# RWKV-style attention and two feed-forward layers on one core: where the decay test and its two small inputs are handled

## The chip, the cores and the metric

The kernel runs on 1 core of a Trainium2 chip. The metric is the device time of one execution in microseconds (us); the figure compared is the median over several runs. The core has a matrix engine (TensorE, PE in the profile), VectorE (DVE), ScalarE (ACT), GpSimd (POOL) and SyncE (SP), each with its own instruction stream; they wait for each other by semaphores. Loads and stores are DMAs, issued by an engine on its own queue and carried out by 16 DMA engines that all queues share. In this kernel SyncE issues all loads, and ScalarE's queue is used for stores only.

## The reference, cut to what matters

Shapes: B=4, H=8, S=768, D=48, so 3072 tokens of width 384. All is float32.

```python
# attention: r, k, v [B,H,S,D]; decay w [H,D]; bonus u [H,D]
for t in range(S):
    cur = einsum('bhd,bhe->bhde', u * k_t, v_t)
    y[t] = einsum('bhd,bhde->bhe', r_t, state + cur)
    state = w * state + einsum('bhd,bhe->bhde', k_t, v_t)
# layer 1 (384 -> 1536 -> 384):  ((x @ w_a) * (x @ w_b)) @ w_out
# layer 2 (384 -> 2048 -> 384):  h = x @ w_in;  (h * clip(h + 3, 0, 6) / 6) @ w_out
```

The inputs have w between 0.85 and 0.95.

## The kernel before, in words

**The whole.** The attention is done in 24 chunks of 128 steps of one batch (`CH = 128`, six tiles of four batches). In a chunk, r and k are multiplied by powers of w and of 1/w, so that the recurrence becomes matrix products. This is safe only for w in a range, 0.75 to 1.33; therefore the kernel tests the range on the chip and holds two complete paths, a fast one and a general one. The four chunks of tile 0 are done in a prologue; all later ones beside the matrix products of layer 1. Then layer 2 follows. The products of both layers are done as three products of high and low parts each (`PRODUCTS`), with weights cut into those parts by ScalarE and GpSimd while TensorE works. The orders of all engines are written out by hand, by slots (`slot_a`, `slot_b`, `slot_d`).

**The prologue, engine by engine.** SyncE (`first_loads`, L387) issues w_u_col (the pairs of w and u, 5 KB), then `first_rk` of chunks 0 to 3 (r and k turned, 512 KB each), then two loads of v. After the flag it goes on with the loads of the fast path (`sync_fast`). VectorE (`guard_and_tables`, L1184) sets `zeros` and the first power, waits for w_u_col, compares w with the lower and the upper bound (L1196, L1198), computes the powers of w by four scans (L1201), then compares the count that TensorE has made (L1204), casts it to the integer flag (L1206), makes the reciprocals (L1208, L1209), waits for `first_rk` of chunk 0 and multiplies its r and k (`first_product`, L1049), makes the table of 1/w powers (L591), and goes on with the chunks (`scale` L1044, `mask` L1067 and L1072). GpSimd sets `three`, makes the masks by eight selects (`make_masks`, L478, the select itself is L487), zeroes the state (L1270) and reads the flag. ScalarE loads its function table with its first activation (L1279), reads the flag, and copies and scales for the chunks (L1002, L854). TensorE multiplies zeros (`keep_warm`, L756, 4 or 2 blocks of 128 columns), sums `in_range` times 3 into the count (L1293), multiplies zeros again (4 blocks and then 2), and begins the chunks (`first_chunks`): `own_of_first` (L630) needs the product of chunk 0, ScalarE's copies (L1002, L854) need `own_of_first`, and VectorE's first mask (L1067) needs ScalarE's copies.

**The flag.** Each engine but TensorE calls `decide`: wait for the flag, read it, branch.

Of the kernel before, what the change touches and what calls it, by code (L numbers as in the profile page):

```python
# [20 lines left out]
ALU = mybir.AluOpType  # L21
ACT = mybir.ActivationFunctionType
AX = mybir.AxisListType

P = 128
# [13 lines left out]
W_MIN, W_MAX = 0.75, 1.33  # L39
# [8 lines left out]
def build(nc, r, k, v, w, u, w_a, w_b, w_out, w_in2, w_out2, rk_turned, natural, w_u_pairs, outT):  # L48
# [11 lines left out]
    NP = H // 2  # L60
    W2 = HP + D
# [17 lines left out]
    with ExitStack() as ctx:  # L79
        def sb(name, shape, dt=F32, of=ctx, align=None):  # L80
            if align:
                return of.enter_context(nc.sbuf_tensor(name, shape, dt, align_bytes=align))
            return of.enter_context(nc.sbuf_tensor(name, shape, dt))
# [5 lines left out]
        acc_ps = ctx.enter_context(nc.psum_tensor("acc_ps", [P, KC, TOK], F32))  # L89
        att_ps = ctx.enter_context(nc.psum_tensor("att_ps", [P, 3, TOK], F32))  # L90
# [16 lines left out]
        with ExitStack() as setup:  # L107

            in_range = sb("in_range", [P, NP], of=setup)
            all_in = sb("all_in", [1, 1], of=setup)  # L110
            inv_fine = sb("inv_fine", [P, NP, FINE + 1], of=setup)
            inv_coarse = sb("inv_coarse", [P, NP, COARSE + 1], of=setup)
            zeros = sb("zeros", [P, CH], of=setup)
            tab_sT = sb("tab_sT", [P, NP, CH], of=setup)
# [5 lines left out]
        flag = sb("flag", [1, 1], I32)  # L120


        with ExitStack() as att:
# [4 lines left out]
            w_u_col = sb("w_u_col", [P, 3, NP], of=att)  # L128
# [12 lines left out]
        s_guard, s_count, s_flag = sem("guard_chain"), sem("in_range_counted"), sem("flag_ready")  # L141
        s_w_u, s_u_all, s_masks = sem("w_and_u_loaded"), sem("u_for_all_loaded"), sem("masks_made")
# [26 lines left out]
        s_three = sem("three_set")  # L169
# [135 lines left out]
        def x_view(tile, z, q):  # L305
            return x_cut[:, tile % 2, z, :, cols_of(q)]

        count_ps = acc_ps[0:1, 1, 0:1]
        HD = H * D
        by_head = lambda x: x.rearrange("s (h d) -> s h d", h=H)  # L310
        A_of = lambda q: first_A[:, q % 2] if 2 <= q < B else A[:, q % 2]
# [73 lines left out]
                         x2T_v[:, :, t * TOK:(t + 1) * TOK]).then_inc(s_x2_loaded, 16)  # L385

        def first_loads(sp):  # L387
            sp.dma_start(w_u_col[0:W2], w_u_pairs).then_inc(s_w_u, 16)
            load_first_rk(sp, 0)
            load_first_rk(sp, 1)  # L390
            load_first_rk(sp, 2)
            load_first_rk(sp, 3)
            load_first_v(sp, 0)
            load_first_v(sp, 1)
# [80 lines left out]
                sp.dma_start(outT_v[:, j, cols], st[:, j, :]).then_inc(s_st, 16)  # L475


        def make_masks(pool):  # L478


            def keep_where(at, rows, column, row, base, times, compare):

                block = masks_sb[rows, at:at + times * MID]
                if times > 1:
                    block = block.rearrange("s (n t) -> s n t", n=times)
                pattern = [[column, MID]] if times == 1 else [[0, times], [column, MID]]
                nc.gpsimd.affine_select(out=block, in_=block, pattern=pattern, compare_op=compare, fill=0.0,  # L487
                                        base=base, channel_multiplier=row).then_inc(s_masks, 1)

            every, low_half, high_half = slice(0, P), slice(0, MID), slice(MID, P)  # L490
            late = 2 * P + MID
            nc.gpsimd.memset(masks_sb[:], 1.0).then_inc(s_ones, 1)
            pool.wait_ge(s_ones, 1)
            keep_where(0, every, 1, -1, 0, 1, ALU.is_equal)
            keep_where(MID, every, 1, -1, MID, 1, ALU.is_equal)
            keep_where(P, every, 1, -1, MID, 1, ALU.is_equal)
            keep_where(P + MID, every, 1, -1, 0, 1, ALU.is_equal)
            keep_where(2 * P, low_half, 1, -1, 0, 1, ALU.is_gt)
            keep_where(late, every, 1, -1, MID, NP // 2, ALU.is_gt)
            keep_where(late + NP // 2 * MID, low_half, 1, -1, 0, NP // 2, ALU.is_gt)  # L500
            pool.wait_ge(s_masks, MASK_PARTS - 1)
            keep_where(2 * P, high_half, 1, -1, 0, 1, ALU.is_gt)
            pool.wait_ge(s_masks, MASK_PARTS)
# [250 lines left out]
        def keep_warm(pe, times, bank=up_ps[:, 1]):  # L754

            pe.matmul(bank[:, 0:times * CH].rearrange("p (n c) -> p n c", n=times), zeros[:],  # L756
                      zeros[:].unsqueeze(1).to_broadcast([P, times, CH]), start=True, stop=True)
# [423 lines left out]
                    if i == 4 and t + 1 < TILES:  # L1181
                        x2_low(dve, t + 1)

        def guard_and_tables(dve):  # L1184

            links = [0]

            def link(ins):
                links[0] += 1
                ins.then_inc(s_set, 1)  # L1190

            link(dve.memset(zeros[:], 0.0))
            link(dve.memset(power[:, :, 0:1], 1.0))
            dve.wait_ge(s_set, links[0])
            dve.wait_ge(s_w_u, 16)
            dve.tensor_scalar(in_range[0:W2], w_col[0:W2], W_MIN, None, ALU.is_ge).then_inc(s_guard, 1)  # L1196
            dve.wait_ge(s_guard, 1)
            dve.scalar_tensor_tensor(out=in_range[0:W2], in0=w_col[0:W2], scalar=W_MAX, in1=in_range[0:W2],  # L1198
                                     op0=ALU.is_le, op1=ALU.mult).then_inc(s_guard, 1)
            for p in range(NP):  # L1200
                link(dve.tensor_tensor_scan(power[0:W2, p, 1:CH + 1], w_col[0:W2, p:p + 1].to_broadcast([W2, CH]),  # L1201
                                            zeros[0:W2, :], 1.0, ALU.mult, ALU.add))
            dve.wait_ge(s_count, 1)
            dve.tensor_scalar(all_in[:], count_ps, 3.0 * W2 * NP - 1.0, None, ALU.is_ge).then_inc(s_guard, 1)  # L1204
            dve.wait_ge(s_guard, 3)
            dve.tensor_copy(flag[:], all_in[:]).then_inc(s_flag, 1)  # L1206
            dve.wait_ge(s_set, links[0])
            link(dve.reciprocal(inv_fine[0:W2], fine[0:W2]))  # L1208
            link(dve.reciprocal(inv_coarse[0:W2], coarse[0:W2]))  # L1209
            first_product(dve, 0)  # L1210
            dve.wait_ge(s_set, links[0])
            table(dve, tab_rk[0:W2, 1, :, 0:CH], inv_coarse[0:W2, :, 0:COARSE],
                  inv_fine[0:W2, :, 1:FINE + 1]).then_inc(s_tabT, 1)
# [37 lines left out]
        def decide(eng):  # L1251
            eng.wait_ge(s_flag, 1)
            return eng.value_load(flag[0:1, 0:1], min_val=0, max_val=1)

        with nc.Block() as block:
            @block.sync
            def _(sp):
                first_loads(sp)
                flag_sp = decide(sp)
                with sp.If(flag_sp == 1):  # L1260
                    sync_fast(sp)
                with sp.Else():
                    sync_general(sp)
                store_last(sp)
                sp.wait_ge(s_st, 16 * (2 * TILES - 1 + KC))
            @block.gpsimd
            def _(pool):
                nc.gpsimd.memset(three[:], 3.0).then_inc(s_three, 1)
                make_masks(pool)
                nc.gpsimd.memset(state[:], 0.0).then_inc(s_zero, 1)  # L1270
                flag_pool = decide(pool)
                with pool.If(flag_pool == 1):
                    pool_fast(pool)
                with pool.Else():
                    pool_general(pool)
            @block.scalar
            def _(act):
                act.wait_ge(s_three, 1)
                nc.scalar.activation(first_use[:], three[:], ACT.Copy)  # L1279
                flag_act = decide(act)  # L1280
                with act.If(flag_act == 1):
                    scalar_fast(act)
                with act.Else():
                    scalar_general(act)
                evacuate_last(act)
            @block.tensor
            def _(pe):
                pe.wait_ge(s_set, 1)
                keep_warm(pe, 4)
                pe.wait_ge(s_three, 1)  # L1290
                pe.wait_ge(s_guard, 2)
                for p in range(NP):
                    mm = pe.matmul(count_ps, in_range[0:W2, p:p + 1], three[0:W2, :], start=(p == 0), stop=(p == NP - 1))  # L1293
                mm.then_inc(s_count, 1)
                keep_warm(pe, 4)
                keep_warm(pe, 2)
                first_chunks(pe)
                tensor_layer1(pe)
                tensor_layer2(pe)
            @block.vector  # L1300
            def _(dve):
                guard_and_tables(dve)
                flag_dve = decide(dve)
                with dve.If(flag_dve == 1):
                    vector_fast(dve)
                with dve.Else():
                    vector_general(dve)
# [172 lines left out]
```

## Time and profile before

| | us |
|---|---|
| median of 3 runs | 919.6 (919.18 to 920.41) |
| profiled execution, device time | 919.12 |
| its span, first to last instruction | 917.3 |
| TensorE busy | 911.9 (99%) |
| VectorE, ScalarE, GpSimd busy | 369.5, 329.5, 184.3 |
| mean granted TensorE clock | 1.00 |

The profiled execution's device time is 1.8 us over its span. Times of instructions are counted from the span's start. An entry "idle before <- X" says what an engine waited for. A start time and a busy time of a merged group do not have to add up to the next start, since neighbours overlap by the engine's pipeline.

### The profile page before, as it was taken

The page shows a single profiled execution, that of the slowest core. Times are in us where ns is not written, and L with a number is a line of the kernel's source. Part 1 is how long each engine was busy: PE and PEld are TensorE (multiplying, and loading weights), DVE is VectorE, ACT ScalarE, POOL GpSimd, SP SyncE. Part 2 cuts the span into 40 slices and gives each one's busy share as a digit, 9 for nine tenths or more (in the row PEclk, how much of TensorE's full clock was granted, in tenths as well). Part 3 has the DMA queues.
Part 4 walks back from the last instruction along what each step waited for, and adds up shares of the span by engine and source line. Part 5 has one row for each costly group of instructions (what it writes and reads, how often), then busy time and mean ns, then how long its engine had stood idle before and what let it go on. Part 6 is the DMA issues. An engine that isn't in the chain of part 4 may idle for free.

```text
span 917.3 us, 15108 instructions
## 1 busy us (share of the span) xinstructions
PE 911.9 (99%) x6400; PEld 746.4 (81%) x6400; DVE 369.5 (40%) x607; ACT 329.5 (36%) x651; POOL 184.3 (20%) x168
## 2 busy tenths in 40 slices
PE   8999999999999999999999999999999999999998
PEld 6788888888888888888888888888888888888887
DVE  7746344525443343334222343343343343343332
ACT  6645323232333233242221343433333333333333
POOL 5976102111111111010755570000000000000000
PEclk9999999999999999999999999999999999999999
DMA  8653211121120121131311210100200100100000
GB/s 307 198 167 108 90 50 62 55 90 56 56 110 34 56 110 55 38 129 48 115 50 55 78 50 1 65 5 1 69 1 0 70 1 7 64 0 1 35 1 36
DMA packets 24281, 57.84 MB, mean 63 GB/s; under 512 B 2320, under 2 KB 8080, under 8 KB 24208
## 3 DMA queue, kind: packets, MB, share of 16 engines
q1 hardware_dynamic: 19808, 48.18, 15.6%
q10 hardware_dynamic: 4400, 8.65, 2.5%
q8 instruction: 50, 0.82, 0.4%
q14 instruction: 23, 0.19, 0.1%
HBM read 47.39 MB, written 9.44 MB: 62 GB/s over the span
## 4 chain that ended last, share of the span: by engine, by line
PE 98%; DVE 1%; DMA 0%; ACT 0%; issue 0%; SPq 0%; DVEq 0%; ACTq 0%
PE up_ps L722 32%; PE up_ps L799 21%; PE acc_ps L736 16%; PE acc_ps L813 11%; PE att_ps L813 11%; PE att_ps L614 2%; PE att_ps L677 1%; PE att_ps L682 1%; PE att_ps L646 1%; PE att_ps L663 1%; PE att_ps L671 1%; DMA first_rk<-in_rk_turned 0%; ACT A L854 0%; DVE first_rk L1044 0%; DVE first_A L1067 0%
## 5 line engine op out<-in xcount | busy, mean ns | idle before, releaser
L722 PE MATMUL up_ps<-x_cut,w_up 128*128 128x512 f32 x1296 | 307.3, 391 | 0.2 <-ACT x_cut L867 0.2
L722 PEld LDWEIGHTS up_ps<-x_cut,w_up 128*128 128x128 f32 x1296 | 241.7, 188 | 52.9 <-issue 3.0
L926 ACT ACTIVATE g_cut<-tmp 128x512 fp32r<-128x512 f32 x168 | 106.2, 632 | 214.4 <-DVE tmp L1149 141.6
L1157 DVE SCALAR_TENSOR_TENSOR g_cut<-tmp,g_cut 128x512 fp32r<-128x512 f32 x168 | 125.2, 745 | 117.5 <-ACT g_cut L926 117.5
L736 PE MATMUL acc_ps<-g_cut,w_down 128*128 128x512 f32 x648 | 157.3, 390 | 0.0
L736 PEld LDWEIGHTS acc_ps<-g_cut,w_down 128*128 128x128 f32 x648 | 121.3, 188 | 26.0 <-issue 0.6
L1151 DVE SCALAR_TENSOR_TENSOR tmp<-tmp,up_ps 128x512 f32<-128x512 f32 x96 | 66.1, 689 | 182.9 <-ACT tmp L920 182.9
L920 ACT ACTIVATE tmp<-up_ps,three 128x512 f32<-128x512 f32 x96 | 66.2, 690 | 171.0 <-PE up_ps L799 171.0
L1149 DVE TENSOR_TENSOR tmp<-tmp,up_ps 128x512 f32<-128x512 f32 x72 | 49.5, 688 | 169.7 <-PE up_ps L722 169.6
L799 PE MATMUL up_ps<-x_cut,w_up 128*128 128x512 f32 x432 | 105.7, 389 | 0.0
L799 PE MATMUL up_ps<-x_cut,w_in_first 128*128 128x512 f32 x432 | 105.4, 389 | 0.0
L799 PEld LDWEIGHTS up_ps<-x_cut,w_up 128*128 128x128 f32 x432 | 81.1, 188 | 16.8
L799 PEld LDWEIGHTS up_ps<-x_cut,w_in_first 128*128 128x128 f32 x432 | 81.1, 188 | 16.8
L918 ACT ACTIVATE tmp<-up_ps 128x512 f32<-128x512 f32 x72 | 43.0, 598 | 112.4 <-PE up_ps L722 112.4
L513 POOL TENSOR_TENSOR nat<-nat 128x384 f32<-128x384 f32 x20 | 23.6, 1180 | 278.9 <-DMA nat<-in_natural 278.9
L813 PE MATMUL att_ps<-g_cut,w_up 128*128 128x512 f32 x324 | 79.3, 389 | 0.0
L813 PE MATMUL acc_ps<-g_cut,w_up 128*128 128x512 f32 x324 | 79.3, 389 | 0.0
L813 PEld LDWEIGHTS att_ps<-g_cut,w_up 128*128 128x128 f32 x324 | 60.8, 188 | 12.6
L813 PEld LDWEIGHTS acc_ps<-g_cut,w_up 128*128 128x128 f32 x324 | 60.8, 188 | 12.6
L854 ACT ACTIVATE A<-masks_sb,own 128x128 f32<-128x128 f32 x160 | 50.3, 388 | 5.6 <-DVE own L1060 5.6
L243 POOL TENSOR_TENSOR w_up<-w_raw,w_up 128x512 fp32r<-128x512 f32 (+2 forms) x42 | 47.3, 1140 | 6.9 <-ACT w_up L237 5.2
L1101 DVE TENSOR_TENSOR x_cut<-att_ps,x_cut 128x384 fp32r<-128x384 f32 x21 | 11.7, 557 | 60.3 <-ACT x_cut L867 60.3
(109 smaller groups left out, 557.2 us busy)
## 6 DMA issues: line engine op xcount, KB each, us to landing
nat<-in_natural SPq DMA_DIRECT2D x20, 704.0 KB, 6.0
rkT<-in_rk_turned SPq DMA_DIRECT2D x20, 512.0 KB, 3.6
w_raw<-in_moe_w_out SPq DMA_DIRECT2D x28, 192.0 KB, 2.4
layer_out_T<-stage ACTq DMA_DIRECT2D x6, 768.0 KB, 3.4
x_cut<-layer_out_T SPq DMA_DIRECT2D x6, 768.0 KB, 4.3
outT<-stage ACTq DMA_DIRECT2D x5, 768.0 KB, 3.3
w_raw<-in_moe_w_in SPq DMA_DIRECT2D x12, 256.0 KB, 4.6
first_rk<-in_rk_turned SPq DMA_DIRECT2D x4, 512.0 KB, 5.6
```

Of the source, the lines that this page charges most:

```text
L243: nc.gpsimd.tensor_tensor(out=pieces[m][1](LO), in0=raw_of(m), in1=pieces[m][1](HI).bitcast(F32), op=ALU.subtract).then_inc(s_w_cut, 1)
L722: mm = pe.matmul(up_ps[:, m, :], w_up[i // PB][:, a, m, c, cols], x_cut[:, t % 2, b, c, :], start=(z == 0), stop=(z == len(order) - 1))
L736: mm = pe.matmul(acc_ps[:, j, :], w_down[:, a, i, j * P:(j + 1) * P], g_cut[:, (t * N1 + i) % GR, b, :], start=(i == 0 and z == 0), stop=( ...
L799: mm = pe.matmul(up_ps[:, i % 2, :], in2_at(a, c, i), x_cut[:, t % 2, b, c, :], start=(c == 0 and z == 0), stop=(c == KC - 1 and z == 2))
L813: mm = pe.matmul(sums(t)[:, j, :], wo2_at(a, i)[:, j * P:(j + 1) * P], g_cut[:, n % GR, b, :], start=(i == 0 and z == 0), stop=(last and z ...
L854: ins = nc.scalar.activation(A_at(q, half)[:, p, :], id_sb[p // 2], ACT.Copy, scale=mine[:, h:h + 1])
L918: nc.scalar.activation(tmp[:, i % 2, :], src, ACT.Copy).then_inc(s_act1, 1)
L920: nc.scalar.activation(tmp[:, i % 2, :], src, ACT.Relu, bias=three[:, 0:1]).then_inc(s_act1, 1)
L926: nc.scalar.activation(g_cut[:, n % GR, HI, :], tmp[:, n % 2, :], ACT.Copy, scale=1.0 if n < TILES * N1 else 1.0 / 6.0).then_inc(s_gh, 1)
L1149: dve.tensor_tensor(out=tm, in0=tm, in1=up_ps[:, 1, :], op=ALU.mult).then_inc(s_g, 1)
L1151: dve.scalar_tensor_tensor(out=tm, in0=tm, scalar=6.0, in1=up_ps[:, n % 2, :], op0=ALU.min, op1=ALU.mult).then_inc(s_g, 1)
L1157: dve.scalar_tensor_tensor(out=lo, in0=tmp[:, n % 2, :], scalar=1.0 if n < TILES * N1 else 1.0 / 6.0, in1=hi.bitcast(F32), op0=ALU.mult, o ...
```

## The change

The range test of w moves from VectorE to GpSimd (three instructions, placed after the fourth of eight mask selects). The count is compared and cast in one activation on ScalarE: Relu(count - (3*112*4 - 1)) written as an integer, so 1 if every entry is in range and 0 otherwise. The constant comes from one more GpSimd memset. The load of w and u is issued by ScalarE as its first instruction instead of by SyncE as its first. The count goes to another PSUM place. TensorE waits for three increments of the guard instead of two and no longer multiplies the 2 blocks of zeros after the 4.

```diff
-        count_ps = acc_ps[0:1, 1, 0:1]
+        count_ps = att_ps[0:1, 0, 0:1]
@@ first_loads(sp)
-            sp.dma_start(w_u_col[0:W2], w_u_pairs).then_inc(s_w_u, 16)
             load_first_rk(sp, 0)
@@ new, called in make_masks after the fourth keep_where
+        def find_in_range(pool):
+            pool.wait_ge(s_w_u, 16)
+            nc.gpsimd.tensor_scalar(in_range[0:W2], w_col[0:W2], W_MIN, None, ALU.is_ge).then_inc(s_guard, 1)
+            nc.gpsimd.tensor_scalar(not_above[0:W2], w_col[0:W2], W_MAX, None, ALU.is_le).then_inc(s_guard, 1)
+            pool.wait_ge(s_guard, 2)
+            nc.gpsimd.tensor_tensor(out=in_range[0:W2], in0=in_range[0:W2], in1=not_above[0:W2],
+                                    op=ALU.mult).then_inc(s_guard, 1)
@@ guard_and_tables(dve), now tables_of_powers(dve)
             dve.wait_ge(s_w_u, 16)
-            dve.tensor_scalar(in_range[0:W2], w_col[0:W2], W_MIN, None, ALU.is_ge).then_inc(s_guard, 1)
-            dve.wait_ge(s_guard, 1)
-            dve.scalar_tensor_tensor(out=in_range[0:W2], in0=w_col[0:W2], scalar=W_MAX, in1=in_range[0:W2],
-                                     op0=ALU.is_le, op1=ALU.mult).then_inc(s_guard, 1)
             for p in range(NP):
                 link(dve.tensor_tensor_scan(...))
-            dve.wait_ge(s_count, 1)
-            dve.tensor_scalar(all_in[:], count_ps, 3.0 * W2 * NP - 1.0, None, ALU.is_ge).then_inc(s_guard, 1)
-            dve.wait_ge(s_guard, 3)
-            dve.tensor_copy(flag[:], all_in[:]).then_inc(s_flag, 1)
@@ gpsimd
                 nc.gpsimd.memset(three[:], 3.0).then_inc(s_three, 1)
+                nc.gpsimd.memset(all_but_one[:], 1.0 - 3.0 * W2 * NP).then_inc(s_three, 1)
@@ scalar
-                act.wait_ge(s_three, 1)
+                act.dma_start(w_u_col[0:W2], w_u_pairs).then_inc(s_w_u, 16)
+                act.wait_ge(s_three, 2)
                 nc.scalar.activation(first_use[:], three[:], ACT.Copy)
+                act.wait_ge(s_count, 1)
+                nc.scalar.activation(flag[:], count_ps, ACT.Relu, bias=all_but_one[:, 0:1]).then_inc(s_flag, 1)
                 flag_act = decide(act)
@@ tensor
-                pe.wait_ge(s_guard, 2)
+                pe.wait_ge(s_guard, 3)
                 ...
                 keep_warm(pe, 4)
-                keep_warm(pe, 2)
```

## Rows read from the trace of the kernel before

**Rows 1.** The page: busy time by engine (share of the span), number of instructions.
```profile
PE 911.9 (99%) x6400; PEld 746.4 (81%) x6400; DVE 369.5 (40%) x607; ACT 329.5 (36%) x651; POOL 184.3 (20%) x168
```

**Rows 2.** TensorE's waits, whole execution: us in total, times, longest.
```profile
PE up_ps L756 <- DVE tab_rk L1193: 1.1, 1, 1.1
...
PE up_ps L722 <- ACT x_cut L867: 0.2, 1, 0.2
```

**Rows 3.** The chain that ended last, 0 to 30 us: start, us, what.
```profile
1.25 3.95 DMA first_rk<-in_rk_turned
...
5.23 0.70 DVE prod L1049
...
5.97 1.06 PE acc_ps L630 x12
...
7.34 2.45 ACT A L854 x8
...
9.91 0.74 DVE A L1067
...
20.55 2.37 PE up_ps L722 x9
```

**Rows 4.** The timeline of all engines: start, us, engine, line, what, [idle before].
```profile
0.80 0.40 SPq L388 DMA_DIRECT2D w_u_col<-in_w_u_pairs  x1
0.80 1.28 ACT L1279 ACT_TABLE_LOAD   x1 [0.80 <-PEq L1433]
...
1.48 1.86 POOL L487 TENSOR_SCALAR_AFFINE_SELECT masks_sb<-masks_sb 128x64 f32<-128x64 f32 x8
...
2.60 0.17 DVE L1196 TENSOR_SCALAR in_range<-w_u_col 112x4 f32<-112x4 f32 x1 [1.52 <-DMA w_u_col<-in_w_u_pairs]
...
2.89 1.36 DVE L1201 TENSOR_TENSOR_SCAN tab_rk<-w_u_col,zeros 112x128 f32<-112x128 f32 x4
3.12 0.34 PE L1293 MATMUL acc_ps<-three,in_range 112*1 112x1 f32 x8
...
4.33 0.14 DVE L1206 CAST flag<-all_in 1x1 int32<-1x1 f32 x1
4.40 0.56 DVE L1208 RECIPROCAL inv_fine<-tab_rk 112x68 f32<-112x68 f32 x1
...
4.88 0.31 DVE L1209 RECIPROCAL inv_coarse<-tab_rk 112x36 f32<-112x36 f32 x1
...
5.40 0.94 SPq L232 DMA_DIRECT2D w_raw<-in_moe_w_a  x2
...
7.13 0.18 ACT L1002 ACTIVATE own_first<-acc_ps 128x8 f32<-128x8 f32 x1 [0.97 <-PE acc_ps L630]
...
9.86 1.28 POOL L531 TENSOR_TENSOR prod<-first_rk 112x512 f32<-112x512 f32 x1 [5.50 <-DVE first_rk L1044]
```

**Rows 5.** DMA issues at 0.8 us and at 1.24 us: KB, us from issue to landing.
```profile
w_u_col<-in_w_u_pairs SPq DMA_DIRECT2D x1, 5.2 KB, 1.7
first_rk<-in_rk_turned SPq DMA_DIRECT2D x1, 512.0 KB, 4.0
```

**Rows 6.** ScalarE's store at 450.81; a load issued at 448.98, another at 451.81.
```profile
450.81 0.37 ACTq L936 DMA_DIRECT2D layer_out_T<-stage  x1
w_raw<-in_moe_w_out SPq DMA_DIRECT2D x1, 192.0 KB, 2.3
w_raw<-in_moe_w_out SPq DMA_DIRECT2D x1, 192.0 KB, 3.0
```

**Rows 7.** TensorE's timeline: the multiplied zeros (PEld: their weight load).
```profile
1.12 2.08 PE L756 MATMUL up_ps<-zeros 128*128 128x512 f32 x2 [1.12 <-DVE tab_rk L1193]
3.39 2.45 PE L756 MATMUL up_ps<-zeros 128*128 128x512 f32 x4
5.25 0.19 PEld L756 LDWEIGHTS up_ps<-zeros 128*128 128x128 f32 x1 [0.50 <-issue]
6.95 1.12 PE L756 MATMUL up_ps<-zeros 128*128 128x512 f32 x2
```

More of the change, by code:

```diff
@@ L109, in build @@
             in_range = sb("in_range", [P, NP], of=setup)
-            all_in = sb("all_in", [1, 1], of=setup)
+            not_above = sb("not_above", [P, NP], of=setup)
+            all_but_one = sb("all_but_one", [1, 1], of=setup)
             inv_fine = sb("inv_fine", [P, NP, FINE + 1], of=setup)
@@ L497, in make_masks @@
             keep_where(P + MID, every, 1, -1, 0, 1, ALU.is_equal)
+            find_in_range(pool)
             keep_where(2 * P, low_half, 1, -1, 0, 1, ALU.is_gt)
@@ L1182, in vector_layer2, with tables_of_powers @@
                         x2_low(dve, t + 1)
-        def guard_and_tables(dve):
+        def tables_of_powers(dve):
             links = [0]
@@ L1301, in _ @@
             def _(dve):
-                guard_and_tables(dve)
+                tables_of_powers(dve)
                 flag_dve = decide(dve)
```

## The prediction

> **What bounds the kernel now.** I read the share of each engine first: TensorE is busy 911.9 of 917.3 us [rows 1], so whatever does not move TensorE moves nothing. Its waits come next: 1.1 us before its first instruction, and in all the products of layer 1 (L722) one wait of 0.2 us [rows 2]; that view has no wait of layer 2. Beyond the prologue TensorE waits for nobody. So a change to the first microseconds counts in one way only: the layer products begin earlier or later than 20.55 us [rows 3], and the whole remainder slides along by the same amount.
>
> The chain of waits says what sets those 20.55 us. It starts with the landing of the first r and k at 1.25 + 3.95 = 5.20 us, then VectorE's product at 5.23, TensorE's sums of it at 5.97, ScalarE's copy at 7.13 and eight scalings from 7.34, VectorE's first mask at 9.91, and VectorE and the others from mask to mask until 20.55 [rows 3, 4]. The timeline shows what the chain hides: VectorE's second reciprocal ends at 4.88 + 0.31 = 5.19 [rows 4], 0.01 us before that landing. Two chains meet at 5.2 us: the load of r and k, and VectorE's work on w. A gain at 5.23 needs both to be shorter. The change touches both.
>
> **VectorE's chain.** Two comparisons go: the scans start when w has landed, at 2.60 and not at 2.89, 0.29 us earlier. After the scans, which end at 2.89 + 1.36 = 4.25, the compare and the cast go; the reciprocal starts at 4.40 [rows 4]. Without them it can start some 0.03 us after the scans (the step that the timeline shows between dependent instructions), so 0.12 us more. Together 0.41: reciprocals at 3.99 and 4.47, the second ends at 4.78, and the product could start at 4.82.
>
> **The load of r and k.** SyncE's first issue is now w, 0.80 to 1.20, and r and k follow at 1.25 [rows 3, 4]. Without w, r and k are issued at 0.80, 0.45 us earlier; with the same 3.95 us they land at 4.75. Everything else on SyncE's queue ahead of the flag moves up by the same 0.45. Both chains then meet again, at 4.75 and 4.78: product at 4.82 in place of 5.23, a gain of 0.41 us, provided that w still lands at about 0.8 + 1.7 = 2.5 us [rows 5].
>
> **The load of w, on ScalarE's queue.** It is issued at 0.80, where ScalarE's table load now starts [rows 4]; an issue on that queue takes 0.37 us [rows 6] (0.40 on SyncE's, rows 4), so the table load moves to about 1.2 and ends at 2.5, with the first activation behind it. ScalarE is needed next for the count, at 3.5 or later: hidden with about 1 us to spare. What is not shown is how w's 5 KB travel when 512 KB of r and k are put on the other queue in the same moment. Lower bound: they land as now, 2.5 us, since they are no more bytes than before (not earlier, for the issue stays at 0.80). Upper bound: they wait for all of r and k of chunk 0 and land at 4.75. I take the lower one, because both are issued together, each has the same latency ahead of its data, and w is a hundredth of the other in bytes. I keep the upper for the range.
>
> The rows that speak against it: the same load of 192 KB took 2.3 us from issue to landing when alone and 3.0 us when issued 1.0 us after a store on ScalarE's queue [rows 6]. So the two queues do share the DMA engines, and the late one pays for the earlier one. The Trainium skill (DMA: Bandwidth & Descriptors, Queues, rings and completion order) states that each DMA engine goes round between queues only at packet borders, after a packet of typically 9 to 17 descriptors. By that rule a share of r and k that is served first is finished before w's share gets its turn; by the opposite reading, w first, nothing is lost. Either order is open when both are issued at 0.80, and the last of 16 shares decides.
>
> **The range test on GpSimd.** Its four first selects end at 1.48 + 4 x 0.23 = 2.41 (1.86 us for eight), so it is free when w lands. The trace has no such comparison on GpSimd. Nearest rows: VectorE's comparison of the same shape, 0.17, and GpSimd's selects, 0.23 each [rows 4]. Lower bound 3 x 0.17, upper bound twice the select, 3 x 0.46 = 1.4. I take 0.23, the same engine: 0.7 us, and the test is ready at 3.3 and not just before the scans' 2.9. TensorE's zeros ahead of the count end at 1.12 + 2.08 = 3.20 [rows 7], so the count starts at 3.35 in place of 3.12 and ends at 3.7. Behind it on TensorE stand the four blocks of zeros, which take 5.25 - 3.39 = 1.86 us until the next ones load [rows 7], so until about 5.5; the two further blocks are gone. TensorE is then free for the sums of the product, due at 4.82 + 0.70 + 0.04 = 5.56 and not 5.97: no loss. With the upper bound the zeros end at 6.2, and the start moves to 6.2, 0.2 later than before. The four other selects and the zeroing of the state behind it on GpSimd move back by 0.7; GpSimd then idles 5.50 us until 9.86 [rows 4], and ScalarE first reads a mask at 7.3: hidden.
>
> **The flag.** It is written at 4.33 + 0.14 = 4.47 now. On ScalarE: count ready at 3.7, one activation of 0.18 (the copy out of PSUM at 7.13, rows 4), about 3.95. SyncE's loads behind the flag move from 5.40 to about 4.9. They feed weights whose lateness TensorE nowhere pays for [rows 2], so this earns nothing. The waiting instruction on ScalarE has only the branch and the fast path behind it, whose first need is at 7.13. The extra memset, about 0.1 us of GpSimd before 1.48, and the new place of the count cost nothing.
>
> **The sum.** 0.41 us earlier at 5.23, handed on through the chain of [rows 3] by the same instructions: sums at 5.56, scalings at 6.93, first mask at 9.50, layer products at 20.14. Against the profiled execution: 919.12 - 0.41 = 918.7. The median of the runs is 0.5 us above that execution, so 919.2 as a median. A measurement of this kernel can tell 0.2%, 1.8 us, from no change: 0.41 us is far below.
>
> **Rivals.**
>
> 1. w lands late (the one that ends on the other side). Place: the wait of the scans for w. From a landing of w at T, the scans start at T + 0.10 and the product at T + 2.33; that passes 5.23 when T is above 2.9, so 0.4 us of lateness decides the sign. At the upper bound, T = 4.75, the product starts at 7.1: 1.9 us later than before, 921.5. In the middle, T = 3.7, it is 0.8 later, 920.4. For it: [rows 6]. Against it: w is small, and issued no later. Most of its span is still within 1.8 us; its far end is not. In that case the test, count and flag are late too, at about 6.3, still ahead of VectorE's need, and TensorE stands idle between its zeros. It might then work at the lower level of its clock: the same product of zeros took 2.08 us as its first work and 1.12 us later [rows 7], a factor near that of 1.2 to 2.4 GHz, while the granted clock reads 1.00 throughout. The sums in the chain (1.06 us, rows 3) would cost as much again: 922.6 with both.
>
> 2. No gain. If the landing of r and k at 5.20 hangs on something other than the issue (the slowest of the DMA engines, say), the product stays at 5.23; or GpSimd's test is at its upper bound. 919.6 to 919.8. For it: 3.95 us is long for 512 KB. Against: the later landings follow their issues.
>
> 3. The table load comes ahead of ScalarE's issue, so that the change doesn't do what it says. w then lands 1.28 us later, at 3.8, and the product starts at 6.1: 0.9 later, 920.5. Against it: the row of the table load bears the line of the activation, behind the new issue in the program.
>
> **How the numbers follow.** The forecast 0.50; w late 0.28 (919.6 to 921.5), with the slower clock besides 0.05 (922.6); no gain 0.12; the table load first 0.05. The likeliest gives 919.2, its own range 918.8 to 919.7. The range for 8 in 10 runs from 918.7, the spread of the runs before below the forecast, to 921.2, into the late w. Slower by over 0.2% means above 921.4: the far end of rival 1 and its clock case, 0.10. Faster by over 0.2% would need 1.8 us where the whole shared start is shorter by 0.45: 0.02. The rest, 0.88, is no change that can be told.
>
> **What would show it.** w_u_col landing 1.7 us after an issue at 0.80 on ScalarE's queue; r and k issued at 0.80; scans from 2.6; reciprocals from 4.0; product at 4.8; the layer products at 20.1. A wait of the scans for w that ends above 2.9 makes the forecast wrong and rival 1 right; a product waiting for r and k at 5.2 shows rival 2; a table load ahead of the issue, rival 3. A count that starts after 4 us would say that GpSimd's three instructions are dear.

## The result and the profile after

The changed kernel takes 925.31 us (median of 6, 923.82 to 926.27) against 919.69 us before (6 runs, 919.18 to 920.41): ratio of the two 1.0060, 95% interval 1.0047 to 1.0073, so 5.6 us slower. The forecast was 919.2 us. The profiled execution is one of 924.30 us with a span of 922.6, 5.3 us above the 917.3 of before.

The timeline of the changed kernel (start, us, engine, line; line numbers are 10 higher than before in the chunk functions), against [rows 4] and [rows 7]:

```profile
0.80 1.81 SPq L361 DMA_DIRECT2D first_rk<-in_rk_turned  x4
0.81 0.41 ACTq L1281 DMA_DIRECT2D w_u_col<-in_w_u_pairs  x1
...
1.12 2.07 PE L766 MATMUL up_ps<-zeros 128*128 128x512 f32 x2 [1.12 <-DVE tab_rk L1203]
1.25 1.28 ACT L1283 ACT_TABLE_LOAD   x1 [1.25 <-PEq L1439]
...
4.85 0.24 POOL L481 TENSOR_SCALAR in_range<-w_u_col 112x4 f32<-112x4 f32 x1 [2.53 <-DMA w_u_col<-in_w_u_pairs]
4.87 1.44 DVE L1207 TENSOR_TENSOR_SCAN tab_rk<-w_u_col,zeros 112x128 f32<-112x128 f32 x4 [3.80 <-DMA w_u_col<-in_w_u_pairs]
5.17 0.23 POOL L482 TENSOR_SCALAR not_above<-w_u_col 112x4 f32<-112x4 f32 x1
5.47 0.20 POOL L484 TENSOR_TENSOR in_range<-in_range,not_above 112x4 f32<-112x4 f32 x1
...
5.82 0.34 PE L1300 MATMUL att_ps<-three,in_range 112*1 112x1 f32 x8 [2.63 <-POOL in_range L484]
...
6.20 0.25 ACT L1286 ACTIVATE flag<-att_ps,all_but_one 1x1 int32<-1x1 f32 x1 [3.45 <-PE att_ps L1300]
6.34 0.58 DVE L1210 RECIPROCAL inv_fine<-tab_rk 112x68 f32<-112x68 f32 x1
```

VectorE now waits 3.80 us for w: before, w was there for its comparison at 2.60 [rows 4], now it lands at 4.8. TensorE stands 2.63 us ahead of the count.

DMA issues of that kernel between 0.5 and 0.85 us (KB each, us from issue to landing), against [rows 5]:

```profile
first_rk<-in_rk_turned SPq DMA_DIRECT2D x1, 512.0 KB, 3.8
w_u_col<-in_w_u_pairs ACTq DMA_DIRECT2D x1, 5.2 KB, 4.0
```

The 5.2 KB take 4.0 us, a little more than the 512 KB beside them. r and k did come earlier, at 4.6 instead of 5.2.

The chain of waits of the changed kernel, 0 to 40 us (start, us, what), against [rows 3]:

```profile
0.81 3.96 DMA w_u_col<-in_w_u_pairs
...
6.16 2.01 PE up_ps L766 x2
8.17 1.38 PE acc_ps L640 x12
9.54 2.01 PE up_ps L766 x2
11.55 1.49 PE up_ps L624 x32
13.04 1.07 PE acc_ps L640 x12
...
14.34 2.46 ACT A L864 x8
...
20.61 1.13 issue
...
25.51 2.34 PE up_ps L732 x9
```

The question is which engine owns this chain. Before, TensorE had one piece ahead of the first masks, 1.06 us. Now it has nearly everything from 6.16 to 14.1: multiplied zeros at 2.01 us for four blocks, which took 1.12 us at 6.95 in [rows 7], and the 32 products of a chunk at 1.49 us. The layer products begin at 25.51, 4.96 us after those of before. From there to the end the two executions need the same within 0.3 us (922.6 - 25.51 = 897.1, 917.3 - 20.55 = 896.8). All but 0.3 us is lost in the first 25 us.

### The profile page after: what moved, and what is told of

Its sections match the earlier page's. It is cut to its first block, busy times and chain, and to the rows that moved or that the text cites. A ratio compares the mean times of both kernels' runs of the same rounds, so it can differ in the third digit from the quotient of the medians.

```text
span 922.6 us, 15103 instructions
## 1 busy us (share of the span) xinstructions
PE 913.6 (99%) x6398; PEld 747.7 (81%) x6398; DVE 369.8 (40%) x603; ACT 329.6 (36%) x652; POOL 184.5 (20%) x172
## 4 chain that ended last, share of the span: by engine, by line
PE 98%; DMA 0%; ACT 0%; DVE 0%; issue 0%; POOL 0%; DVEq 0%
PE up_ps L732 32%; PE up_ps L809 21%; PE acc_ps L746 16%; PE acc_ps L823 11%; PE att_ps L823 11%; PE att_ps L624 2%; PE att_ps L687 1%; PE att_ps L692 1%; PE att_ps L656 1%; PE att_ps L673 1%; PE att_ps L681 1%; PE up_ps L766 0%; DMA w_u_col<-in_w_u_pairs 0%; ACT A L864 0%; PE acc_ps L640 0%
```

## Experiments

Each runs on one chip in turn with the kernel before, which had medians of 919.4 to 919.6 us there. A difference in us is taken against that median of the same session. The times of most changed kernels spread more than those of the kernel before, and often fall into groups, so the groups are given. "A pause" is time in which TensorE does nothing, and "zeros" are the multiplied zeros of `keep_warm`.

**e1: w back on SyncE's queue.** The changed kernel with

```diff
         def first_loads(sp):
+            sp.dma_start(w_u_col[0:W2], w_u_pairs).then_inc(s_w_u, 16)
 ...
-                act.dma_start(w_u_col[0:W2], w_u_pairs).then_inc(s_w_u, 16)
```

> The changed kernel with the load of w and u put back as SyncE's first issue; the range test stays on GpSimd, the flag on ScalarE, the two blocks of zeros stay out. Theory Q (the 5.6 us come from w travelling on ScalarE's queue beside 512 KB of r and k, with TensorE's idle time and slow clock as its consequence): w lands at about 2.5 us again instead of 4.8, count at 3.4, first product of VectorE at about 5.2 and the first layer product at about 20.5; 919.2 to 920.0 us in all. Rival G (the moved range test, the flag or the missing zeros cost by themselves, since they stand in TensorE's way): at least 1.5 us stay, 921 us or more, with the count starting after 4 us or TensorE's sums (12 matmuls) taking 1.6 us and not 1.04.

Measured: 923.13 us (10 runs; five at 920.98 to 921.92, four at 924.34 to 924.63, one at 926.58), ratio 1.0034 (1.0022 to 1.0045). The median lies in the gap between two groups. Theory Q fell in its plain form: the load is in its old place and 3.7 us of the median remain. Rival G's forecast came true, in the total and in the sums. Its timeline, in a profiled execution of 926.58 us, the slowest of the ten:

```profile
2.67 0.24 POOL L482 TENSOR_SCALAR in_range<-w_u_col 112x4 f32<-112x4 f32 x1 [0.34 <-DMA w_u_col<-in_w_u_pairs]
...
3.64 0.34 PE L1300 MATMUL att_ps<-three,in_range 112*1 112x1 f32 x8 [0.45 <-POOL in_range L485]
3.90 2.07 PE L767 MATMUL up_ps<-zeros 128*128 128x512 f32 x2
...
5.01 0.69 DVE L1060 TENSOR_TENSOR prod<-first_rk 112x512 f32<-112x512 f32 x1
...
5.77 1.73 PE L641 MATMUL acc_ps<-w_u_col,prod 112*128 112x64 f32 x12
```

VectorE's product is 0.22 us earlier than before, as forecast for the part that VectorE hands over. But TensorE's 12 sums take 1.73 us in place of 1.04 to 1.06. The chain of this execution, 0 to 34 us:

```profile
7.50 2.01 PE up_ps L767 x2
9.51 1.49 PE up_ps L625 x32
11.00 1.67 PE acc_ps L641 x12
12.66 1.49 PE att_ps L625 x32
...
21.70 1.49 PE att_ps L625 x32
...
27.71 2.37 PE up_ps L733 x9
```

The same instructions last 1.6 to 1.8 times as long, up to about 25 us, with TensorE at work without a break from 3.64 us on; the layer products begin at 27.71. The row of this stretch (us; busy us of PE, PEld, DVE, ACT, POOL; then the granted clock, 1.00) and its counterpart of before show that the clock column does not tell the two apart:

```profile
8.00:16.00 8.00, 8.00 (x86) 5.80 (x84) 4.63 (x7) 4.89 (x17) 2.53 (x2) 1.00 1.06 384
```

```profile
8.00:16.00 8.00, 7.50 (x186) 6.30 (x188) 7.51 (x11) 7.61 (x28) 2.93 (x3) 1.00 1.04 385
```

86 matmuls in 8 us against 186. The zeros, 2.01 us against 1.12, are near the factor between the two levels, 1.2 and 2.4 GHz. Why the column reads 1.00 all the same is told behind h1.

**e2: only the load moved.** The kernel before, with the load of w issued by ScalarE as its first instruction and SyncE's taken out.

> The kernel before with only the load of w and u moved to ScalarE's queue. Theory Q: w lands at 4.7 to 4.8 us, the scans start 2 us late, the count at 5.3, VectorE's first product at about 7.4 (its compare and flag are still in its way), TensorE slow as in the changed kernel: 923.5 to 926 us. Rival G: 1.9 us at the most, so 919.6 to 921.5 us.

Measured: 926.53 us (5 runs: 922.04, 922.23, 926.53, 926.88, 927.19), ratio 1.0065 (1.0043 to 1.0087). The median is 0.5 us above theory Q's range of 923.5 to 926, and far above rival G's 921.5; single executions lie on both sides of Q's range. In its profiled execution (922.23) the DMA row reads 0.81 + 4.00, so w lands at 4.8 again, and TensorE idles 2.2 us ahead of the count. The load alone is enough for more than the whole loss (7.1 us); e1 says that the other parts without it are enough for 3.7. So the parts are not a sum: both open a way to the same loss.

**e3: TensorE kept at work until the count.** The changed kernel, w still late, with

```diff
                 keep_warm(pe, 4)
+                keep_warm(pe, 4)
+                keep_warm(pe, 2)
                 pe.wait_ge(s_three, 1)
                 pe.wait_ge(s_guard, 3)
```

> The changed kernel, w still on ScalarE's queue, with 4 + 2 more blocks of multiplied zeros on TensorE ahead of the count, so that it works from 1.1 to about 5.9 us without a pause. Theory C (beyond the 1.85 us by which the first product is late, the rest is TensorE at the lower level of its clock after the idle 3.2 to 5.8 us): zeros behind the count take 1.1 us instead of 2.0, the 12 sums 1.04 instead of 1.58, the first mask comes at about 11.8 instead of 13.2; 921.2 to 922.5 us. Rival D (the rest is the late landing itself, handed on through VectorE and ScalarE, and the pause of 1.1 us at 20.6): no change, 924 to 926 us.

Measured: 921.16 us (10 runs, 920.75 to 921.35), ratio 1.0016 (1.0006 to 1.0025). Theory C holds (the median 0.04 us below its range, the sums at the 1.04 us it named), rival D falls. TensorE's timeline:

```profile
1.12 4.63 PE L766 MATMUL up_ps<-zeros 128*128 128x512 f32 x6 [1.12 <-DVE tab_rk L1203]
5.82 0.34 PE L1302 MATMUL att_ps<-three,in_range 112*1 112x1 f32 x8
6.09 1.47 PE L766 MATMUL up_ps<-zeros 128*128 128x512 f32 x2
7.75 1.04 PE L640 MATMUL acc_ps<-w_u_col,prod 112*128 112x64 f32 x12 [0.19 <-DVE prod L1059]
```

w lands at 4.8 and the count starts at 5.82, as in the changed kernel; the only difference is useless work in the pause, and 3.9 us of the 5.6 us and nearly all of the spread are gone. What is left, 1.7 us, is the late landing by itself: the layer products begin at 22.32, 1.8 us after those of before.

**e4: SyncE held back by 0.7 us.** The changed kernel with SyncE waiting for GpSimd's memset of the masks before its first load, so that it issues at 1.48 us, 0.67 us after w.

```diff
         def first_loads(sp):
+            sp.wait_ge(s_ones, 1)
```

> The changed kernel with SyncE's first issue held until GpSimd has set the mask buffer (1.41 us): w leaves 0.65 us ahead of r and k, still on ScalarE's queue. If the two transfers alternate packet by packet because both are there from the start (theory Q), w now lands at 2.5 us, r and k at about 5.4, the first product at 5.45: 919.6 to 920.3 us. If ScalarE's queue is slow for a load as such (rival S), w still lands after 3.5 us and the time stays at 922 us or more.

Measured: 921.87 us (5 runs: 920.95, 921.48, 921.87, 924.19, 924.47), ratio 1.0035 (1.0021 to 1.0049). The landing is as theory Q had it; the total is not, since the count still came after a pause (3.20 to 3.49 us), which I had left out of this expectation. The issues before 1.6 us:

```profile
first_rk<-in_rk_turned SPq DMA_DIRECT2D x1, 512.0 KB, 3.5
w_u_col<-in_w_u_pairs ACTq DMA_DIRECT2D x1, 5.2 KB, 1.6
```

ScalarE's queue carries w in 1.6 us if r and k come 0.67 us later. Rival S, a queue that is slow as such, falls.

**f1: the two blocks of zeros back, in e1.** The kernel e1 with `keep_warm(pe, 2)` behind the four again.

> The changed kernel with w loaded first on SyncE's queue (as e1), and the two further blocks of multiplied zeros back behind the count. e1 showed TensorE at half speed for most of the prologue in its slow executions. Theory P (what holds it slow is the pause ahead of the later count, 3.2 to 3.6 us, after which its work counts anew): the two blocks help only partly and cost time behind the count, so the executions still differ by 2 us or more and the median is 920.5 to 924 us. Rival Z (the missing two blocks alone: there is a pause between the zeros and the sums): 919.2 to 920.0 us, and all executions within 1 us.

Measured: 924.79 us (10 runs; three at 919.35 to 919.87, seven at 924.65 to 926.79), ratio 1.0049 (1.0031 to 1.0066). Above the range of theory P, on its side; Z alone falls. This kernel differs from the one before in the place of the test and the flag only, and TensorE's pause ahead of the count is 0.3 us (the count at 3.51). It is either as good as the kernel before or 5 us worse. It multiplies as many blocks of zeros as the kernel before, so their number alone does not decide.

**f2: the two blocks out, in the kernel before.**

> The kernel before with only the two blocks of zeros behind the four taken out; its count comes without a pause, at 3.12 us, and TensorE is idle from about 5.4 to 5.97. Theory P: no cost, 919.3 to 919.8 us. Rival Z: TensorE is slow for part or all of the prologue, 921 us or more, with executions that differ by over 2 us.

Measured: 921.16 us (10 runs; four at 918.89 to 919.37, three at 921.03 to 922.10, three at 924.40 to 924.92), ratio 1.0025 (1.0009 to 1.0042). Theory P as I had put it is wrong here, and rival Z's forecast came true: there is no pause ahead of the count in this kernel, and it is a matter of chance all the same. Its profiled execution is one of the good ones (919.02); the pause it has is behind the zeros, 5.14 to 5.82:

```profile
3.12 0.34 PE L1293 MATMUL acc_ps<-three,in_range 112*1 112x1 f32 x8
3.39 1.75 PE L756 MATMUL up_ps<-zeros 128*128 128x512 f32 x2
5.82 1.04 PE L630 MATMUL acc_ps<-w_u_col,prod 112*128 112x64 f32 x12 [0.68 <-DVE prod L1049]
```

So either pause will do: one ahead of the count (f1) or one ahead of the sums (f2).

**f3: e1 with one block of zeros ahead of the count.**

> The changed kernel with w loaded first on SyncE's queue, and one more block of zeros ahead of the count, which fills 3.20 to 3.63 us, so that the count at 3.64 follows without a pause; four blocks behind it, the two stay out. Theory P: TensorE reaches its full speed as in the kernel before, first product at 5.0, layer products at 20.3; 919.2 to 919.6 us, all executions within 1 us. Rival Z: still 921 us or more.

Measured: 919.05 us (10 runs; eight at 918.73 to 919.33, two at 921.10 and 921.15), ratio 1.0002 (0.9993 to 1.0012). Rival Z falls. One block, 0.43 us of useless work, takes 4 us off e1's median. But "all within 1 us" was wrong: two of ten still fall in the middle group; the pause ahead of the sums (0.52 us) is still there.

**f4: w on ScalarE's queue with a small lead, and one block ahead.** As f3, but w on ScalarE's queue, and SyncE waits for GpSimd's first two memsets, so that it issues at 0.94.

> The changed kernel, w on ScalarE's queue, SyncE's first issue held for the two small memsets of GpSimd (about 0.9 to 1.0 us), and one more block of zeros ahead of the count. If w needs to be ahead of r and k by the 0.2 us only, it lands at about 2.5, r and k at about 4.9, the first product starts at 4.9, and with theory P the time is 919.0 to 919.4 us. If 0.2 us is not enough of a lead, w lands after 3 us, the count comes after a pause, and the time is 921 us or more.

Measured: 920.96 us (10 runs; three at 918.91 to 919.00, six at 920.78 to 921.49, one at 923.85), ratio 1.0014 (1.0003 to 1.0025). w landed 1.9 us after its issue at 0.81, between the two cases that I had put, so a lead of 0.13 us is nearly enough; the count at 3.77 came after a short pause again (the zeros end at 3.62).

**g1 and g2: no pause at all.** g1 is f3 with the two blocks back behind the count. g2 is f4 with two blocks ahead instead of one.

> The changed kernel with w loaded first on SyncE's queue, one more block of zeros ahead of the count (as in the kernel f3) and the two blocks of zeros back behind it: TensorE has no pause from 1.1 us to the sums at about 5.9 us. Theory P2 (any pause before the sums, ahead of the count or behind the zeros, leaves it to chance whether TensorE gets its full speed in the prologue; without one it always does): all executions within 1 us, median 918.9 to 919.4 us. Rival R (the moved range test or flag make it a matter of chance in another way): some executions at 921 us or above, as 2 of 10 in f3.

> The changed kernel, w on ScalarE's queue, SyncE's first issue held until about 0.94 us, two more blocks of zeros ahead of the count and four behind it. f4, with one block ahead and a pause of about 0.15 us, ran at 918.9 to 923.9 us. Theory P2: w lands at 2.7, the first product starts at 5.0, TensorE works through to about 5.9; all executions within 1 us, 919.0 to 919.5 us. Rival R: executions at 921 us or above remain.

Measured: g1 919.60 us (11 runs, 918.94 to 920.42), ratio 0.9999 (0.9990 to 1.0008): nothing above 920.5, as theory P2 says, where f1, with one block less, had seven of ten at 924.65 or more, and rival R falls; its median is over the range, that of the kernel before being 919.62 in the same session. g2 918.93 us (11 runs, ten at 918.54 to 919.45 and one at 921.31), ratio 0.9993 (0.9984 to 1.0002): P2 said "always", and one run is against it. The kernel before itself had one run at 921.59 of 21 here, so a rest of chance is there without a visible pause too. g2 is the fastest kernel of the study, by 0.7 us at the median, but its interval holds 1: no proven gain.

**h1: twice the packets.** The kernel e3 with a second copy of w and u, into an unused buffer, ahead of w on ScalarE's queue (the flag waits for it as well).

```diff
+                act.dma_start(stage[0:W2, 0:3 * NP].rearrange("d (a b) -> d a b", a=3), w_u_pairs).then_inc(s_copy, 16)
                 act.dma_start(w_u_col[0:W2], w_u_pairs).then_inc(s_w_u, 16)
```

> The kernel e3 (w on ScalarE's queue beside r and k, TensorE kept at work until the count) with a second copy of the 5 KB of w and u, into an unused buffer, issued ahead of w on ScalarE's queue; so each DMA engine has 14 packets of 48 bytes there in place of 7, and the one that matters is issued 0.4 us later. Theory A (a DMA engine with both queues waiting takes one packet from each in turn, so each small packet costs one 4 KB packet of r and k): the copy lands at about 4.7 us as w did, and w at 5.7 to 6.5 us, about when r and k of chunk 1 land; first product at about 8.3, 922 to 923 us. Rival B (a whole transfer from each queue in turn, w behind r and k of chunk 0): w lands at 4.8 to 5.2 us, 921.2 to 921.6 us.

Measured: w lands at 5.98 us and the first product starts at 8.28, as theory A says; rival B's 4.8 to 5.2 us falls. In all it is 927.16 us (4 runs: 924.10, 927.15, 927.18, 927.58), 4 us above the expectation. The zeros of e3 end at 5.75 and the count now comes at 7.03, so the pause is open again, and in the profiled execution of 924.10 us the loss with it:

```profile
1.25 4.73 DMA w_u_col<-in_w_u_pairs
...
7.03 0.34 PE att_ps L1305 x8
7.37 2.00 PE up_ps L767 x2
```

(The chain of this kernel: start, us, what.) The three others list a mean granted clock of 0.993 where this one has 1.00; no trace shows what their 3 us more are. The packets in the traces fit the alternation. Started packets of both queues, by size, in quarters of a us, in the changed kernel:

```
us       SyncE's queue     ScalarE's queue
2.25     4096 B x13        48 B x2
2.50     4096 B x19        48 B x16
2.75     4096 B x14        48 B x15
3.00     4096 B x19        48 B x19
3.25     4096 B x25        48 B x24
3.50     4096 B x23        48 B x24
3.75     4096 B x26        48 B x8
4.00     4096 B x28        48 B x4
```

The two queues start nearly as many packets as each other while both last. The traces do not say which of the 16 DMA engines carried a packet, so that each engine alternates is an inference from these counts and from h1. Each engine has 7 of the small (112 rows on 16 engines) and 8 large per chunk of r and k; a small one takes about 0.01 us, most of the large ones 0.16 and some up to 0.46. In h1 the 48 B packets run on until 5.25 to 5.5.

The alternation is not the whole delay. In e1, first on SyncE's queue, the 48 B packets start from 1.81 to 2.20 us and w lands at 2.59. In the changed kernel they start from 2.47 to 4.24: 0.66 us of the 2.2 us more is a later first packet, which nothing here explains, and 1.4 us is the longer stretch.

**When TensorE gets its full speed.** The packed traces hold a record of the granted clock (two levels, 1.2 and 2.4 GHz), and its first entry, 1.00 of full speed, does not start with the kernel. What lies before it the clock column fills in as 1.00. The start of that entry, for the profiled execution of each run (f2's trace has no entry):

```
kernel    execution, us    full speed from, us
before    919.12            5.23
f3        919.33            4.67
g1        919.18            5.34
g2        919.33            6.06
f1        919.61            6.75
e4        920.95           10.26
f4        921.35           10.53
e1        926.58           25.52
e3        921.17            6.82   (w late)
e2        922.23            9.87   (w late)
changed   924.30           13.15   (w late)
h1        924.10           13.48   (w at 5.98)
```

The durations agree: in f4 the zeros at 7.42 still take 2.08 us, the 32 products at 9.43 take 1.40, between 1.56 and 0.90, and the next 12 sums, at 10.76, take 1.04. So the change of speed can be placed in each execution, and with w on time it orders the totals: 4.67 to 6.75 gives 919.1 to 919.6, about 10.4 gives the middle group, 25.52 the slowest execution of all.

## Why the prediction was wrong

**Right.** TensorE bounds the kernel, only the start of the layer products counts, and the chain behind them carries any shift one to one: the rest from there on was 896.8 to 897.1 us in the kernel before, the changed one, e1 and e3. ScalarE's issue is ahead of its table load, which moved to 1.25 and is hidden (rival 3 falls). r and k came 0.6 us earlier, so their landing follows their issue (rival 2 falls). GpSimd's test took 0.20 to 0.24 us an instruction, 0.83 us in all (4.85 to 5.68), 0.1 more than the 0.7 taken. The flag on ScalarE took 0.25 us and is in no chain. The gain of 0.41 us at the first product appeared in no run. In the variants of the changed kernel that have w on time the product starts at 4.93 (g1) to 5.12 us (f3), 0.1 to 0.3 us earlier than before; there r and k were issued at 0.94 us or later.

**The step that failed first: "I take the lower one"**, for the landing of w at 2.5 us. It landed at 4.77; the upper bound was 4.75. The reason given (same latency, a hundredth of the bytes) was about bytes; h1 shows that packets count, since 112 more of 48 bytes ahead of w put its landing at 5.98. Rival 1 had place and price right: product at 7.08 (7.1 at its upper bound), and 1.85 us late. e3 gives the price in the total, 1.7 us. Of the order, the text had "a share of r and k that is served first is finished before w's share gets its turn", which by itself would also give a landing near 4.8; h1 and the packet counts speak for turns packet by packet instead. The Trainium skill (DMA: Bandwidth & Descriptors, Queues, rings and completion order) has the round robin at packet borders, as seen here, but with a packet of typically 9 to 17 descriptors; here the counts fit a change-over after every row of 4096 or 48 bytes.

**The step that failed most: the slow clock as an appendix of rival 1, at 1.1 us and a chance of 0.05**, and with it "the two further blocks are gone ... no loss". Measured, it is worth 3.9 of the 5.6 us (e3), 5 us in f1's slow group, and up to 7.2 us (e1's slowest execution, whose layer products begin at 27.71 with w on time). Two things were missed. First, its size: I charged only the 12 sums. While TensorE runs at half speed, the zeros behind the count stand in the way of the sums too (6.16 to 8.17 us, while the product was done at 7.7), the zeros between sums and products of chunk 0 take 2.01 us, and the 32 products of a chunk 1.49; then TensorE, not VectorE, carries the chain. The multiplied zeros are cover while TensorE is fast, and a queue in front of the real work while it is slow. Second, its condition: I tied it to a late w. But 0.3 us ahead of the count (f1) or the two missing blocks (f2) bring it about with w on time. The zeros had been charged as filler; without a pause in them TensorE gets its full speed in time (g1, eleven of eleven). [rows 7] had the sign: 2.08 us for the first four blocks, 1.12 for the same work at 6.95, so the change-over lies between (the trace has it at 5.23), and the change took work out of just this stretch.

The Trainium skill (TensorE: Matmul & The Clock Gate, Part 1: The HAM clock gate) says that TensorE's clock is throttled by default, that activity releases it, and that the moment varies from run to run because the monitor does not start with the kernel. The groups of f2 (918.9 to 919.4, 921.0 to 922.1, 924.4 to 924.9), made by one program, agree with the last point. The second point e1 does not bear out so plainly: TensorE worked there from 3.64 us without a break and got its full speed only at 25.52.

**How the 5.3 us of the profiled execution divide.** 1.8 us late w (22.32 - 20.55, by e3). 3.2 us slow TensorE (25.51 - 22.32): in it a stop of 1.13 us at 20.61 under "issue", with TensorE at full speed since 13.15, so this stop is not the slow clock. A shorter one lies in the chain at the same 32 products in f3 (0.34 us) and f2 (0.10 us). 0.3 us behind 25.5 is unexplained.

**Left open.** What the 1.13 us are (waiting for instructions is possible, not shown). What sets the moment of full speed: the runs show that a pause lets it slip, not by what rule, and e1's 25.52 least of all. The middle group is the one with full speed from about 10.4 us (e4, f4); the group 5 us above the lowest was never caught in a profile with w on time. That a pause ahead of the count and one behind the zeros work in the same way is an inference from the spreads of f1, f2, f3 and g1.

## What to carry to other kernels

Before a tiny load that others wait for is moved to a second queue, count its packets per DMA engine and ask what is issued in the same moment: each may have to wait for one large packet of the neighbour, and a lead of some tenths of a us, or the old queue, avoids it. Filler work on TensorE at the start is part of the critical path as long as TensorE is slow: look at the duration of the same matmul early and late, not at the clock column, and keep the filler without a pause until the first real work. When runs of one kernel fall in groups some us apart, take ten of them before judging a change of half a us.

## What was not expected of the hardware

- 5.2 KB on a second queue took 4.0 us beside 512 KB (e2 the same), 1.6 us with 0.67 us of lead, 1.9 with 0.13, 1.6 to 1.8 first on the same queue; behind a copy of itself 4.7.
- With a pause of 0.3 us on TensorE (f1) seven of ten executions were 5 us slower; with one block of zeros in its place (g1) all eleven were at 920.42 or less.
- TensorE stayed slow through 21.9 us of unbroken work (e1, from 3.64 to 25.52 us; the 32 products took 1.56 us at 21.64, in place of 0.90).
- The record of the granted clock begins only with the full speed (4.67 to 25.52 us after the start), so a mean of 1.00 does not exclude a slow start.
